# Layer 1 of the first two blocks in 256-token sets beside more attention, and all loops written out

## The chip, the cores and the metric

One Trainium2 chip, one core of it. The metric is the device time of the whole program in microseconds (us), from one launch. The engines are TensorE (PE; its weight loads are listed apart as PEld), VectorE (DVE), ScalarE (ACT), GpSimd (POOL), and SyncE (SP), which issues all transfers here. Work in PSUM is done in eight banks of 512 float32 columns.

## The reference

An attention with a decaying state, then two feed-forward layers. B = 4, H = 8, S = 768, D = 48; 3072 tokens of 384 values; d_ff is 1536 in layer 1 and 2048 in layer 2.

```python
for t in range(S):
    kt, vt, rt, wt = (k[:, :, t], v[:, :, t], r[:, :, t], w[:, :, t])
    cur = np.einsum('bhd,bhe->bhde', u[None] * kt, vt)
    y[:, :, t] = np.einsum('bhd,bhde->bhe', rt, state + cur)
    state = wt[:, :, :, None] * state + np.einsum('bhd,bhe->bhde', kt, vt)
...
gate = 1.0 / (1.0 + np.exp(-(x @ w_gate)))
val = x @ w_val
x = gate * val @ w_out
...
h = x @ w_in
g = np.where(h > 0.0, h, alpha * (np.exp(np.minimum(h, 0.0)) - 1.0))
out = g @ w_out
```

## The kernel before

The 768 time steps are six blocks of 128 (NB = 6), each of all four sequences, so of 512 tokens (TOK). Attention of a block is done in two halves (HALF), of two sequences each; q = 2n + hf numbers the twelve halves. A half goes through twelve stages (STAGES): transposes of w, k and r (Tw, Tk, Tr), six levels L1 to L6 at which the decays of ever longer runs are multiplied in, a transpose of k (KT), the output Y and the new state S. Each stage is two parts (b = 0, 1), one for each sequence, so a half has 24 parts. At a level TensorE multiplies (L544) what VectorE (`next_level_r`, L828) and GpSimd (`next_level_k`, L456) scaled for it; levels 1 to 3 have a masked copy on VectorE (L853), level 4 two sums (L861, L865), and levels 4 to 6 copies on ScalarE. The part of level i for sequence b waits for `next_level_r` of level i - 1 for the same b. The parts take the three banks 5 to 7 in turn, each waiting until the use three back has been read (`bank_free`). When both halves of a block have Y, a step XT transposes the result (L581), and ScalarE and VectorE copy it as a rounded high part xh and a low part xl (L888).

Layer 1 multiplies in three passes (high by high, high by low, low by high), in units called thirds. For each of the F1 = 12 tiles of d_ff there are the groups g (gate), v (value) and o (output), of three thirds each; a third is three matmuls (L606 for g and v, L615 for o) of 128 rows by 512 columns, in all 324 a block. After g ScalarE takes the sigmoid (L716); after v VectorE makes the product h (L907), ScalarE copies it rounded (hh, L669) and VectorE takes the rest (hl, L897), which o needs. The last two o groups (LATE) stand at the end.

The order is the same list for all engines, which each walk it in order. Block 0's attention comes first, alone (`FIRST`). Then `MIXED` is walked for n = 0 to 4: layer 1 of block n, with the 48 parts of block n + 1 spread over its 102 thirds, at the end XT of block n + 1 and LATE. For n = 1 to 4 it is a loop of the engines. `LAST` is layer 1 of block 5 alone. Then layer 2 follows for the six blocks (L631, L639), a loop too; it reads the result of layer 1 from a scratch in device memory (`store_x2`, `load_x2`).

The weights of layer 1 are 36 pieces of 128 x 384. Each is loaded into a ring of four (`raw_w1`, NR1), then ScalarE copies it rounded (L669, WS<-work) and VectorE takes the rest (L917); this is `split_w1`. Six are split in the second half of block 0 (`EARLY`), one more after each third third of layer 1 of block 0, until all 36 are. A group g waits for its tile's three pieces. SyncE's queue is in order: it waits for the ring, and for nat (w, k, r of a half) until level 4 of the half before has been done with it (`load_half` waits on d_shift).

Of the kernel before, what the change touches and what calls it, by code (L numbers as in the profile page):

```python
# [13 lines left out]
def build(nc, r, k, v, w, u, w_gate, w_val, w_out, w2_in, w2_out, out):  # L14
# [41 lines left out]

    def use_of(hf, name, i):

        return (HALF * ATT if name == "XT" else hf * ATT + 2 * STAGES.index(name)) + i

    def nth(hf, name, i):

        return use_of(hf, name, i) + 1

    ORDER = [(hf, name, i) for hf in range(HALF) for name in STAGES for i in range(2)] + \
            [(0, "XT", i) for i in range(KC)]
    AT = {use_of(*x): x for x in ORDER}

# [6 lines left out]
    THIRDS = [(*group, i) for group in GROUPS for i in range(3)]  # L75
    LATE = [("o", j, i) for j in (F1 - 2, F1 - 1) for i in range(3)]
    PARTS = [("a", hf, name, b) for hf in range(HALF) for name in STAGES for b in range(U)]
    XT = ("a", 0, "XT", 0)
    MIXED = []
    for i, third in enumerate(THIRDS):  # L80
        MIXED.append(third)
        MIXED += [PARTS[s] for s in range(len(PARTS)) if s * (len(THIRDS) - 3) // len(PARTS) == i]
    MIXED += [XT] + LATE
    FIRST = PARTS + [XT]
    LAST = THIRDS + LATE

    N1 = 3 * F1
    AHEAD = 6
    EARLY = [len(FIRST) // 2 + 10 + 2 * x for x in range(AHEAD)]
# [12 lines left out]
    with ctx:  # L102
# [35 lines left out]
        NR1 = 4  # L138
        raw_w1 = work[:, 0:NR1 * KC * P].rearrange("p (n f) -> p n f", n=NR1)
# [18 lines left out]
        w1_loaded = [sem(f"w1_loaded{i}") for i in range(NR1)]  # L158
        w2_loaded = [sem(f"w2_loaded{i}") for i in range(NR)]
        x2_stored, out_stored = sem("x2_stored"), sem("out_stored")  # L160
# [57 lines left out]
        def attn_bank(hf, name, i):  # L218
            return ATTN + use_of(hf, name, i) % NBK
# [791 lines left out]
```

## Time and profile before

| | |
|---|---|
| median of 3 runs | 1202.69 us (1201.72 to 1202.88) |
| the profiled execution, its span | 1203.3 us |
| PE busy | 1155.1 us, 96% |
| PEld busy | 1006.2 us, 84% |
| DVE busy | 669.5 us, 56% |
| ACT busy | 472.2 us, 39% |
| POOL busy | 295.5 us, 25% |
| block 0's attention, up to its XT | 90.8 us |
| layer 1 of block 0 with attention of block 1, XT to XT | 133.6 us |
| the same for later blocks | 121.8 us each |

A busy PE is not PE at its peak: a matmul's recorded length overlaps the next one's, so distances between starts tell its price. A weight load runs beside the matmul before it. "Idle before" of a row is how long that engine waited and for whom.

### The profile page before, as it was taken

How to read it: one execution, taken by the hardware profiler on the slowest of the kernel's cores; microseconds unless marked ns; L12 is line 12 of the kernel's file. 1: busy time of each engine (PE TensorE's matmuls, PEld its weight loads, DVE VectorE, ACT ScalarE, POOL GpSimd, SP SyncE). 2: the span in 40 equal slices, each digit the busy share in tenths (PEclk: the TensorE clock that was granted, in tenths of full speed). 3: DMA queues.
4: the chain of work that ended last, by engine and by line, in shares of the span. 5: the costliest groups of instructions: out<-in, count | busy, mean ns of one | idle time of the engine just before them, and what ended most of it. 6: DMA issues, size and time to landing. Idle time of an engine off the chain costs nothing.

```text
span 1203.3 us, 18133 instructions
## 1 busy us (share of the span) xinstructions
PE 1155.1 (96%) x6336; PEld 1006.2 (84%) x6336; DVE 669.5 (56%) x1044; ACT 472.2 (39%) x889; POOL 295.5 (25%) x290
## 2 busy tenths in 40 slices
PE   5778998999999999999999999999999999999999
PEld 4666777888888888888888888889999899899998
DVE  8777868494839393939393933354433334343433
ACT  2433444333333333333333333365544545454543
POOL 5563434143615351535153520000000000000000
PEclk9879998999999999999999999999999999999999
DMA  5451624122312231133204004220100101010000
GB/s 85 80 95 44 106 65 86 40 37 30 54 40 27 38 48 43 20 45 39 53 12 54 0 19 138 66 71 23 52 0 12 40 0 52 0 52 0 26 0 26
DMA packets 153413, 51.80 MB, mean 43 GB/s; under 512 B 126624, under 2 KB 148768, under 8 KB 153376
## 3 DMA queue, kind: packets, MB, share of 16 engines
q1 hardware_dynamic: 153376, 51.33, 21.0%
q8 instruction: 20, 0.33, 0.1%
q14 instruction: 17, 0.14, 0.0%
HBM read 41.88 MB, written 9.44 MB: 43 GB/s over the span
## 4 chain that ended last, share of the span: by engine, by line
PE 82%; DVE 11%; issue 4%; ACT 2%; DMA 0%; POOL 0%; DVEq 0%; SPq 0%; POOLq 0%; ACTq 0%
PE ps L606 21%; PE ps L639 17%; PE ps L631 16%; PE ps L615 10%; PE ps L544 7%; DVE RKW L828 6%; PE ps L560 3%; PE ps L534 3%; PE ps L565 2%; PE ps L573 2%; DVE hl L897 1%; DVE A L853 1%; DVE WS L917 1%; ACT RKW L669 1%; PE ps L581 1%
## 5 line engine op out<-in xcount | busy, mean ns | idle before, releaser
L606 PE MATMUL ps<-xh,WS 128*128 128x512 f32 x864 | 251.3, 408 | 1.6 <-DVE xl L888 1.6
L669 ACT ACTIVATE hh<-work 128x512 fp32r<-128x512 f32 x168 | 106.4, 633 | 287.5 <-DVE work L907 205.5
L544 PEld LDWEIGHTS ps<-RKW 128*128 128x128 f32 x1152 | 157.2, 203 | 59.1 <-DVE RKW L828 38.8
L544 PE MATMUL ps<-RKW 128*128 128x128 f32 x1152 | 167.6, 293 | 34.2 <-DVE RKW L828 34.0
L639 PE MATMUL ps<-WS,hh 128*128 128x384 f32 x768 | 198.0, 339 | 0.5 <-DVE hl L897 0.5
L828 DVE TENSOR_TENSOR RKW<-RKW,WL 64x256 f32<-64x256 f32 x288 | 186.1, 646 | 16.1 <-PE ps L544 13.7
L606 PEld LDWEIGHTS ps<-xh,WS 128*128 128x128 f32 x864 | 155.1, 190 | 30.7 <-issue 1.8
L897 DVE TENSOR_TENSOR hl<-work,hh 128x512 fp32r<-128x512 f32 x168 | 133.0, 791 | 85.3 <-ACT hh L669 84.3
L631 PE MATMUL ps<-xh,WS 128*128 128x512 f32 x576 | 164.2, 397 | 0.0
L615 PE MATMUL ps<-hh,WS 128*128 128x512 f32 x432 | 161.6, 411 | 0.4 <-DVE hl L897 0.3
L934 DVE SCALAR_TENSOR_TENSOR work<-work,ps 128x512 f32<-128x512 f32 x96 | 66.0, 688 | 172.2 <-ACT work L757 172.2
L456 POOL TENSOR_TENSOR RKW<-RKW,WL 128x256 f32<-128x256 f32 x144 | 111.0, 771 | 189.1 <-PE ps L544 189.1
L639 PEld LDWEIGHTS ps<-WS,hh 128*128 128x128 f32 x768 | 140.8, 188 | 8.7 <-DVE hl L897 1.0
L639 PE MATMUL ps<-WS,hl 128*128 128x384 f32 x384 | 129.9, 338 | 0.0
L606 PE MATMUL ps<-xl,WS 128*128 128x512 f32 x432 | 129.1, 407 | 0.0
L631 PEld LDWEIGHTS ps<-xh,WS 128*128 128x128 f32 x576 | 107.4, 188 | 18.8
L716 ACT ACTIVATE work<-ps 128x512 f32<-128x512 f32 x72 | 43.1, 599 | 155.8 <-PE ps L606 155.0
L755 ACT ACTIVATE work<-ps 128x512 f32<-128x512 f32 x96 | 57.2, 596 | 115.3 <-PE ps L631 115.3
L615 PEld LDWEIGHTS ps<-hh,WS 128*128 128x128 f32 x432 | 81.7, 189 | 17.3 <-DVE hl L897 1.3
L669 ACT ACTIVATE RKW<-ps 128x512 f32<-128x512 f32 (+1 forms) x120 | 70.9, 594 | 53.2 <-PE ps L534 52.8
L669 ACT ACTIVATE A<-ps 16x128 f32<-16x128 f32 (+2 forms) x168 | 57.9, 345 | 82.5 <-PE ps L544 81.0
L907 DVE TENSOR_TENSOR work<-work,ps 128x512 f32<-128x512 f32 x72 | 49.5, 688 | 72.6 <-PE ps L606 48.8
(67 smaller groups left out, 1324.7 us busy)
## 6 DMA issues: line engine op xcount, KB each, us to landing
nat<-in_w_dram SPq DMA_DIRECT2D x24, 192.0 KB, 3.7
nat<-in_k_dram SPq DMA_DIRECT2D x24, 192.0 KB, 4.8
nat<-in_r_dram SPq DMA_DIRECT2D x24, 192.0 KB, 5.2
V<-in_v_dram SPq DMA_DIRECT2D x24, 192.0 KB, 4.5
x_scratch<-work SPq DMA_DIRECT2D x6, 768.0 KB, 3.5
nat<-x_scratch SPq DMA_DIRECT2D x6, 768.0 KB, 5.2
out_dram<-Yt SPq DMA_DIRECT2D x5, 768.0 KB, 3.9
RKW<-in_moe_w_in_dram SPq DMA_DIRECT2D x16, 192.0 KB, 2.4
```

Of the source, the lines that this page charges most:

```text
L456: gp.tensor_tensor(Kb[:, :, :, 0, :], Kb[:, :, :, 0, :], Wb[:, :, :, 1].to_broadcast([P, PR, P // (2 * L), L]), ALU.mult).then_inc(p_k, 1)
L544: last = mm(bank[b][:, p * P:(p + 1) * P].rearrange("p (e i l) -> p e i l", e=2, l=L), K[:, g, :], Rb[:, :, :, 1, :], start=True, stop=True)
L606: last = mm(ps[:, VAL if val else GATE, :], gate_w(a, val, j, c), xp[b][:, c, :], start=(i == 0 and c == 0), stop=(i == 2 and c == KC - 1))
L615: last = mm(ps[:, ACC + i, :], down_w(a, j, i), hp[b][:, j % 2, :], start=(j == 0 and at == 0), stop=(j == F1 - 1 and at == 2))
L631: last = mm(ps[:, UP2 + j % 4, :], up2_w(a, j, c), xp[b][:, c, :], start=(i == 0 and c == 0), stop=(i == 2 and c == KC - 1))
L639: last = mm(ps[:, ACC2 + b, 0:HD], hp[ap][:, j % 2, b * P:(b + 1) * P], down2_w(wp, j), start=(j == 0 and i == 0), stop=(j == F2 - 1 and i ...
L669: return nc.scalar.activation(o, i, ACT.Copy)
L755: nc.scalar.activation(sig, ps[:, UP2 + j % 4, :], ACT.Relu, scale=-1.0).then_inc(a_relu, 1)
L828: last = tt(out_R, Rb, Wb[rows, :, :, 0].to_broadcast([HP, PR, P // (2 * L), L]), ALU.mult)
L897: tt(hl[:, j % 2, :], h, f32(hh[:, j % 2, :]), ALU.subtract).then_inc(d_lo, 1)
L907: tt(h, sig, ps[:, VAL, :], ALU.mult).then_inc(d_h, 1)
L934: nc.vector.scalar_tensor_tensor(h, sig, -1.0, ps[:, UP2 + j % 4, :], ALU.add, ALU.max).then_inc(d_elu, 1)
```

## The change

Layer 1 of blocks 0 and 1 is done in four sets of 256 tokens (two sequences, one half), the later blocks as before; `SETS` lists them, `cols(m)` gives a set's columns of the 512 in every tile and bank. A set 0 needs only half 0 of block 0, so its transposes (`transpose_x`, 6 for 12) stand after half 0, and half 1 of block 0 runs beside set 0. `STREAM` is all attention with the transposes, `PROGRAM` the whole order. Beside set 0 go the 24 parts of half 1 and the transposes for set 1; beside set 1 all 24 parts of half 2, the transposes and 8 parts of half 3 (`MORE`); beside set 2 the other 16, the transposes, and 16 of half 4; beside set 3 the other 8, half 5 whole and the transposes of block 2. From there the order is the former one.

A matmul of layer 1 in these sets has 256 columns for 512, so there are twice as many, 648 a block; the operations of ScalarE and VectorE on sig, h, hh, hl, xh, xl and x2 have 256 columns too and are twice as many. The six early weight pieces are split at levels 5, 6 and KT of half 0, the other 30 in set 0, again one after each third third. The first eight pieces are loaded ahead of half 1's inputs, two into unused space behind the ring and two into the idle half of Yt; after that the ring has four places. All loops are written out. Banks are given by the place of a use in `USES`; `x2_stored` is one semaphore a half.

```diff
+    HALVED = 2
+    TH = U * P
+    SETS = [(n, (hf,)) for n in range(HALVED) for hf in range(HALF)] + [(n, (0, 1)) for n in range(HALVED, NB)]
+    NS = len(SETS)
+    MORE = {1: 8, 2: 16}
+    def cols(m):
+
+        return slice(SETS[m][1][0] * TH, (SETS[m][1][-1] + 1) * TH)
...
+    PROGRAM = STREAM[:STREAM.index(("x", 0)) + 1]
+    done = len(PROGRAM)
+    phase = {}
+    for m in range(NS):
+        beside = STREAM[done:STREAM.index(("x", m + 1)) + 1 + MORE.get(m, 0)] if m + 1 < NS else []
+        done += len(beside)
+        phase.update({step: m for step in beside})
+        if beside and beside[-1][0] == "x" and SETS[m + 1][1] == (0, 1):
+            PROGRAM += spread(THIRDS[m], beside[:-1], len(THIRDS[m]) - 3) + [beside[-1]] + LATE[m]
+        else:
+            PROGRAM += spread(THIRDS[m], beside, len(THIRDS[m]) - 1) + LATE[m]
...
-    AHEAD = 6
-    EARLY = [len(FIRST) // 2 + 10 + 2 * x for x in range(AHEAD)]
+    EARLY = [("a", 0, name, b) for name in ("L5", "L6", "KT") for b in range(U)]
+    AHEAD = len(EARLY)
...
+        NR1, ONCE = 4, 4
+        raw_w1 = work[:, 0:(NR1 + 2) * KC * P].rearrange("p (n f) -> p n f", n=NR1 + 2)
+        raw_w1_y = Yt[:, G:2 * G].rearrange("p (n q) e d -> p n (q e d)", n=2)
...
-                    if x >= NR1:
-                        sp.wait_ge(d_wlo, x - NR1 + 1)
-                    dst = raw_w1[:, x % NR1, :]
+                    if x >= NR1 + ONCE:
+                        sp.wait_ge(d_wlo, x - (NR1 + ONCE if x < 2 * NR1 + ONCE else NR1) + 1)
+                    dst = w1_raw(x)
...
+            at = [2 * NR1 + ONCE] + [min(N1, NR1 + split_until(("a", 1, name, 1))) for name in ("L4", "Y")] + [N1]
             load_w1(at[0], at[1])
-            load_half(1, 1)
-            load_v(1, 1)
+            load_half(2)
+            load_v(2)
             load_w1(at[1], at[2])
...
+            def transpose_x(m):
+                n, halves = SETS[m]
+                pe.wait_ge(d_y, 2 * (HALF * n + halves[-1] + 1))
+                for c in range(KC):
+                    bank_free("x", m, c)
+                    for b in range(halves[0] * U, (halves[-1] + 1) * U):
+                        last = nc.tensor.transpose(ps[:, bank_of("x", m, c), b * P:(b + 1) * P],
+                                                   o_sb[:, b, c * P:(c + 1) * P], ident[:])
+                    last.then_inc(s_att, 1)
...
                     for c in range(KC):
-                        last = mm(ps[:, VAL if val else GATE, :], gate_w(a, val, j, c), xp[b][:, c, :],
+                        last = mm(ps[:, VAL if val else GATE, t], gate_w(a, val, j, c), xp[b][:, c, t],
                                   start=(i == 0 and c == 0), stop=(i == 2 and c == KC - 1))
...
-            with pe.Fori(1, NB - 1) as i:
-                mixed(i)
-            for step in LAST:
-                layer1(NB - 1, *step)
-            with pe.Fori(0, NB) as i:
+            for step in PROGRAM:
+                if step[0] == "a":
+                    attention(*step[1:])
+                elif step[0] == "x":
+                    transpose_x(step[1])
+                else:
+                    layer1(*step[1:])
+            for n in range(NB):
                 for step in STEPS2:
-                    layer2(i, *step)
+                    layer2(n, *step)
```

TensorE's order where layer 1 begins. Before, after both halves (L573 is S, L581 the transposes to x, L534 Tw and Tk of block 1):

```order
L573 MATMUL ps<-V,RKW 128x96 x8
L581 MATMUL ps<-ident,Yt 128x128 x12
L606 MATMUL ps<-xh,WS 128x512 x3
L534 MATMUL ps<-ident,nat 128x128 x4
L606 MATMUL ps<-xl,WS 128x512 x3
L606 MATMUL ps<-xh,WS 128x512 x3
L534 MATMUL ps<-ident,nat 128x128 x4
```

Now, after half 0 alone (L588 is S, L532 the transposes, L550 Tw of half 1 of block 0, L614 the gate and value matmuls):

```order
L588 MATMUL ps<-V,RKW 128x96 x8
L532 MATMUL ps<-ident,Yt 128x128 x6
L614 MATMUL ps<-xh,WS 128x256 x3
L550 MATMUL ps<-ident,nat 128x128 x4
L614 MATMUL ps<-xl,WS 128x256 x3
L614 MATMUL ps<-xh,WS 128x256 x6
L614 MATMUL ps<-xl,WS 128x256 x3
L550 MATMUL ps<-ident,nat 128x128 x4
```

The transposes to x moved ahead by one half, and a part stands after every four thirds instead of after every second one.

VectorE's order at levels 1 and 2 beside the first layer-1 work. Before, in block 1 (L828 `next_level_r`, L853 the masked copy, L897 the low part, L917 a weight split):

```order
L828 TENSOR_TENSOR RKW<-RKW,WL 64x4x32x2 x2
L853 COPY_PREDICATED A<-masks,ps 128x256x2
L897 TENSOR_TENSOR hl<-work,hh 128x512
L917 TENSOR_TENSOR WS<-work,WS 128x384
L828 TENSOR_TENSOR RKW<-RKW,WL 64x4x32x2 x2
L853 COPY_PREDICATED A<-masks,ps 128x256x2
L828 TENSOR_TENSOR RKW<-RKW,WL 64x4x16x4 x2
L853 COPY_PREDICATED A<-masks,ps 128x128x4
```

Now, in half 1 beside set 0 (L817, L842, L888, L909 are the same four, L899 the product h):

```order
L817 TENSOR_TENSOR RKW<-RKW,WL 64x4x32x2 x2
L842 COPY_PREDICATED A<-masks,ps 128x256x2
L909 TENSOR_TENSOR WS<-work,WS 128x384
L817 TENSOR_TENSOR RKW<-RKW,WL 64x4x32x2 x2
L842 COPY_PREDICATED A<-masks,ps 128x256x2
L899 TENSOR_TENSOR work<-work,ps 128x256
L909 TENSOR_TENSOR WS<-work,WS 128x384
L888 TENSOR_TENSOR hl<-work,hh 128x256
L909 TENSOR_TENSOR WS<-work,WS 128x384
L817 TENSOR_TENSOR RKW<-RKW,WL 64x4x16x4 x2
L842 COPY_PREDICATED A<-masks,ps 128x128x4
```

Between level 1 and level 2 of the first sequence there were one split and one layer-1 operation; now there are three splits and two layer-1 operations of half the width.

## Rows read from the trace of the kernel before

**Rows 1.** The page: busy, 40 slices in tenths, and the chain by engine.

```profile
PE 1155.1 (96%) x6336; PEld 1006.2 (84%) x6336; DVE 669.5 (56%) x1044; ACT 472.2 (39%) x889; POOL 295.5 (25%) x290
DVE  8777868494839393939393933354433334343433
...
PE 82%; DVE 11%; issue 4%; ACT 2%; DMA 0%; POOL 0%; DVEq 0%; SPq 0%; POOLq 0%; ACTq 0%
```

**Rows 2.** Windows by stage: length, busy PE PEld DVE ACT POOL, PEclk, DMA, GB/s.

```profile
48.50:90.83 42.33, 31.07 (x194) 28.13 (x193) 34.65 (x57) 14.79 (x34) 23.92 (x23) 0.80 0.43 74
90.83:224.46 133.63, 122.25 (x705) 102.50 (x704) 100.82 (x158) 52.12 (x112) 49.59 (x46) 0.97 0.36 71
224.46:346.29 121.83, 120.71 (x721) 103.93 (x720) 78.06 (x127) 41.43 (x86) 48.51 (x46) 1.00 0.23 40
```

**Rows 3.** Windows, the six levels of halves 0, 2, 3 and 4.

```profile
15.50:39.71 24.21, 16.94 (x96) 15.73 (x97) 22.70 (x36) 4.95 (x15) 14.27 (x15) 0.86 0.26 44
...
106.94:141.21 34.27, 29.99 (x172) 24.38 (x173) 30.29 (x51) 12.92 (x32) 15.99 (x17) 1.00 0.38 72
168.59:205.96 37.37, 32.48 (x172) 27.11 (x171) 32.78 (x51) 13.59 (x33) 16.07 (x17) 0.91 0.43 80
241.69:271.26 29.57, 29.10 (x172) 24.52 (x171) 27.84 (x42) 9.82 (x24) 15.06 (x17) 1.00 0.31 41
```

**Rows 4.** Timeline of PEld: start, length of the group, form, count.

```profile
748.01 1.36 PEld L606 LDWEIGHTS ps<-xh,WS 128*128 128x128 f32 x6
749.42 0.66 PEld L606 LDWEIGHTS ps<-xl,WS 128*128 128x128 f32 x3
...
902.35 0.19 PEld L639 LDWEIGHTS ps<-WS,hl 128*128 128x128 f32 x1
...
904.11 0.60 PEld L631 LDWEIGHTS ps<-xh,WS 128*128 128x128 f32 x3
...
86.28 1.87 PEld L560 LDWEIGHTS ps<-V,A 128*128 128x128 f32 x16
...
88.07 0.97 PEld L565 LDWEIGHTS ps<-ST,RKW 128*128 128x128 f32 x8
```

**Rows 5.** Timeline at the ends of half 0, of block 0, and at block 2's first dense matmul.

```profile
48.48 1.78 PE L534 MATMUL ps<-ident,nat 128*128 128x128 f32 x12
...
90.72 0.91 PEld L581 LDWEIGHTS ps<-ident,Yt 128*128 128x128 f32 x8
90.83 1.72 PE L581 MATMUL ps<-ident,Yt 128*128 128x128 f32 x12
...
94.13 0.94 PE L606 MATMUL ps<-xh,WS 128*128 128x512 f32 x3 [1.58 <-DVE xl L888]
...
351.82 0.86 PE L606 MATMUL ps<-xh,WS 128*128 128x512 f32 x3
```

**Rows 6.** Timeline in block 1's first half, levels 1 and 2, with releasers.

```profile
110.12 0.56 DVE L917 TENSOR_TENSOR WS<-work,WS 128x384 fp32r<-128x384 f32 x1 [1.11 <-ACT WS L669]
...
112.78 0.97 PEld L544 LDWEIGHTS ps<-RKW 128*128 128x128 f32 x8 [1.39 <-DVE RKW L828]
```

**Rows 7.** Groups by form, block 2's layer 1 (346.29 to 468.12), VectorE and ScalarE.

```profile
L893 DVE TENSOR_TENSOR WL<-RKW 128x512 f32<-128x512 f32 x2 | 1.4, 692 | 8.6 <-ACT RKW L669 8.6
L893 DVE TENSOR_TENSOR WL<-WL 128x256 f32<-128x256 f32 x2 | 0.8, 424 | 0.1
...
L669 ACT ACTIVATE A<-ps 32x256 f32<-32x256 f32 x8 | 3.0, 375 | 2.6 <-PE ps L544 2.6
```

**Rows 8.** A window of L917 alone, half 2's levels; its group, 90.83 to 224.46.

```profile
106.94:141.21 34.27, 5.95 (x9) 1.00 0.38 72
...
L917 DVE TENSOR_TENSOR WS<-work,WS 128x384 fp32r<-128x384 f32 x30 | 22.4, 750 | 17.6 <-ACT WS L669 17.5
```

**Rows 9.** Timeline of SyncE's issues around the loads of a half.

```profile
134.11 0.99 SPq L244 DMA_DIRECT2D nat<-in_w_dram  x2
...
141.47 1.11 SPq L280 DMA_DIRECT2D work<-in_moe_w_val_dram  x1
```

More of the change, by code:

```diff
@@ L74, in build, with spread, splits @@
         GROUPS += [("g", j), ("v", j)] + ([("o", j - 1)] if 1 <= j < F1 - 1 else [])
[L75 to L85, printed above, removed]
-    N1 = 3 * F1
-    AHEAD = 6
-    EARLY = [len(FIRST) // 2 + 10 + 2 * x for x in range(AHEAD)]
+    THIRDS = [[("d", m, *group, i) for group in GROUPS for i in range(3)] for m in range(NS)]
+    LATE = [[("d", m, "o", j, i) for j in (F1 - 2, F1 - 1) for i in range(3)] for m in range(NS)]
+    def spread(dense, parts, room):
+        steps = []
+        for i, third in enumerate(dense):
+            steps.append(third)
+            steps += [parts[s] for s in range(len(parts)) if s * room // len(parts) == i]
+        return steps
+    PROGRAM = STREAM[:STREAM.index(("x", 0)) + 1]
[9 more added lines that the diff above has]
+            PROGRAM += spread(THIRDS[m], beside, len(THIRDS[m]) - 1) + LATE[m]
+    assert done == len(STREAM)
+    N1 = 3 * F1
+    EARLY = [("a", 0, name, b) for name in ("L5", "L6", "KT") for b in range(U)]
+    AHEAD = len(EARLY)
+    def splits(step):
+        return step in EARLY or (step[:2] == ("d", 0) and step[-1] == 2)
+    SPLIT1 = {step: x for x, step in enumerate([step for step in PROGRAM if splits(step)][:N1])}
+    SPLIT2 = {("d", NS - 1, "v", j + 1, 2): j for j in range(F1 - 2)}
+    assert len(SPLIT1) == N1
     DOWNS = F2 - 1 + B
@@ L332, in _ @@
-            load_shift(v, 1, 0)
+            load_v(0)
+            load_shift(v, 0)
+            load_w1(0, NR1 + ONCE)
+            load_half(1)
+            load_v(1)
+            load_w1(NR1 + ONCE, 2 * NR1 + ONCE)
+            load_shift(k, 1)
+            load_shift(v, 1)
             def split_until(step):
-                return AHEAD + sum(x[0] != "a" and x[-1] == 2 for x in MIXED[:MIXED.index(step)])
-            at = [NR1 + AHEAD] + [NR1 + split_until(("a", hf, name, 1)) for hf, name in ((0, "L4"), (0, "Y"), (1, "L4"))] + [N1]
+                return sum(PROGRAM.index(x) < PROGRAM.index(step) for x in SPLIT1)
@@ L374, in _ @@
                 load_w2(j)
-            store_x2(NB - 1)
-            sp.wait_ge(x2_stored, 16 * (NB + 1))
-            with sp.Fori(0, NB - 1) as i:
-                load_x2(i + 1)
-                store_out(i)
+            store_x2(NS - 1)
+            for n in range(NB - 1):
+                load_x2(n + 1)
+                store_out(n)
             for b in range(B):
@@ L705, in attention, with transpose_x, layer1 @@
                         last.then_inc(a_rp, 1)
-                elif name == "XT":
-                    for c in range(KC):
-                        act.wait_ge(s_att, ATT_BLK * n + nth(hf, name, c))
-                        copy(xh[:, c, :], ps[:, attn_bank(hf, name, c), :]).then_inc(a_xhi, 1)
-            def layer1(n, kind, j, third):
+            def transpose_x(m):
+                t = cols(m)
+                for c in range(KC):
+                    act.wait_ge(s_att, count("x", m, c))
+                    copy(xh[:, c, t], ps[:, bank_of("x", m, c), t]).then_inc(a_xhi, 1)
+            def layer1(m, kind, j, third):
+                t = cols(m)
                 if third < 2:
```

473 lines of the change are left out of this document (197 added, 276 removed).

## The prediction

> **What bounds the kernel now.** I read the busy row and the slices first [rows 1]: TensorE is busy 96% of the span, and VectorE, 56% in all, is at seven to eight tenths in the first seven slices (some 210 us). The chain is 82% TensorE and 11% VectorE [rows 1]. The windows by stage show why [rows 2]: from 48.50 to 90.83 us, the second half of block 0 alone, TensorE shows work for 31 of 42 us; the block that follows (layer 1 of block 0 with attention of block 1) takes 133.63 us, and the next 121.83 us, with TensorE busy 120.71. That gives two things to win: the 42.3 us in which the second half stands alone, and the 11.8 us by which the first mixed block is longer.
>
> What the waits are is seen in the windows over the six levels of one half [rows 3]. In the half that runs first (15.50 to 39.71) they take 24.21 us with VectorE busy 22.70. In block 1's two halves they take 34.27 and 37.37 us with VectorE busy 30.29 and 32.78; in the first of block 2's 29.57, where TensorE is busy 29.10. So levels are VectorE's while weights are being split, and just about even later.
>
> **The price of a matmul.** Busy times of matmuls overlap, so I take the distance between starts of weight loads, one per matmul [rows 4]. 512 columns: six loads from 748.01, the next at 749.42, 0.235 each; over a long stretch 0.232. 384 columns: ten from 902.35 to 904.11, 0.176. Attention's float32 ones of 48 columns (each runs as two instructions): sixteen from 86.28 to 88.07, 0.112; its matmuls of 128 columns also stand at 0.112 (eight loads end 0.97 after the first starts [rows 6]). From 512 to 384 the step is 0.056 per 128 columns, so **256 columns cost 0.176 - 0.056 = 0.120**, a price that before has no row for. Its bounds: 0.112, the pace of the shortest pairs (gain), and 0.190, the mean duration of one weight load, if each had to end before the next matmul. I take 0.120, since the 48-column loads also last 0.19 [rows 4] and follow at 0.112.
>
> With these, TensorE's own work is: one half of attention, 32 transposes at 0.109 (eight from 90.72 show 0.91 [rows 5]) and 160 other executed pairs (96 of levels, 64 of the Y and S stages) at 0.112, 21.4 us; layer 1 of a block, 324 matmuls, 75.2 us at 512 columns and 2 x 324 x 0.120 = 77.8 us in two sets; so 38.9 us a set and **+2.6 us a block, +5.2 us** in all. A transpose step to the next layer is 0.65 us for a set and 1.3 us for a block.
>
> **Up to the first set.** The half alone ends at 48.48 [rows 5]. Six weight pieces are now split at its levels 5, 6 and KT, which stood in the second half before. Six splits of 0.56 [rows 6] would be 3.3 us, if VectorE were the bound throughout; it is busy 94% of the levels [rows 3], but the stage KT, where two of the six fall, waits for others. So between 2.2 and 3.3, and little is certain of the two: I take 2.3, and 50.8. From the transposes to the first dense matmul were 94.13 - 90.83 = 3.3 us [rows 5]; with six transposes for twelve (-0.65) and copies of 256 columns (0.42 for 0.69 on VectorE [rows 7], as much again on ScalarE), 2.2 us: first dense matmul at 53.0.
>
> **Set 0, with the second half and 30 splits beside.** TensorE's work is 38.9 + 21.4 + 0.65 = 61.0 us. The code puts a half's 24 parts over 101 thirds of layer 1, so the six levels (12 parts) span 48.5 thirds: 48.5 x 3 x 0.120 + 12 x 0.896 = 28.2 us of TensorE. VectorE in the same stretch: attention alone 22.7 us in the half alone [rows 3]; in half 2 30.29 less nine splits of 5.95 [rows 8] and six products and low parts of 0.69, 20.2; I take 21.7. Sixteen splits, one after every third third, at 0.69, between 5.95/9 = 0.66 and the group's mean of 0.750 [rows 8]: 11.0. Five products and five low parts at 0.42 and 0.46 (a 256-column operation is 0.424 where 512 take 0.692, ScalarE's 256-element copy 0.375 [rows 7]): 4.7. Each split behind a product waits for ScalarE, which copies h first and the weight piece second; before, 1.11 us [rows 6], now 0.85 with the shorter copy, times 5.4: 4.6. Other idle 0.7. Sum **42.7 us against 28.2: +14.5 us**. The same sum gives before's 34.27 (30.29 busy + 3.3 on ScalarE + 0.7). The three transpose stages ahead come to 14 us against 11.4; one part's lead absorbs some: +1.8. KT, Y and S (16.8 us of TensorE, 12.8 of VectorE) hide everything. Set 0 is 77.3 us, and ends at 130.3.
>
> **Sets 1 to 3, with 1.33 halves each.** TensorE's work is 3 x 38.9 + 4 x 21.4 + 2 x 0.65 + 1.3 = 204.9 us. Parts stand 3.06 thirds apart, so six levels are 24.0 us of TensorE. VectorE has 21.7 + 3.6 (eight layer-1 operations) + 1.5 idle as in the half alone = 26.8: +2.9 a half. Bounds: 25.3 with no idle (+1.4), and 25.3/0.88 = 28.8 (+4.8), 0.88 being busy over length in block 1's levels [rows 3]. The masked levels and level 4 have the most work in a row, so I take 3.5, **+14 us** for four halves. Three banks go round, and a transpose step is followed by the next T after three thirds (1.1 us) where before the late down projections stood between: about 0.5 us twice and 0.5 at the first whole block, +1.5.
>
> **The sum.** The first dense matmul of block 2 stood at 351.82 [rows 5]; after that the order is before's, unrolled. Now: 53.0 + 77.3 + 204.9 + 14 + 1.5 = 350.7. Difference -1.1 us. In the profiled execution that is 1203.3 - 1.1 = 1202.2; its span stands 0.6 us over the median 1202.69, so 1201.6. Loops gone: a pass of the loop has TensorE busy 120.71 of 121.83 us [rows 2], and the levels' waits make up most of the rest, so nothing is counted. The saved 42.3 us are eaten by 21.4 + 0.65 of work that must still be done, 5.2 of shorter matmuls, 2.3 of splits and some 13 to 16 of waits beyond the former.
>
> **TensorE's rule.** The rows show 0.232 for 512 columns and 0.176 for 384 [rows 4]. The Trainium skill (TensorE: Matmul & The Clock Gate, Back-to-back issue gap) gives 262 cycles for 256 columns, 0.109 us at 2.4 GHz. By that the price would be below mine and at the attention pairs' floor; it is the third rival. The same table gives 518 cycles, 0.216, for 512, which the trace contradicts by 0.016.
>
> **The rivals.**
> First, slower: VectorE's levels in sets 1 to 3 behave like block 1's (0.88 busy at the higher density, waits falling between in-order operations) and set 0's splits take their mean of 0.750 [rows 8]: 4 x (4.8 - 3.5) = 5.2, 16 x 0.06 = 1.0, and the three heavy levels and level 4 (4.4, 4.4, 4.4, 4.8 of VectorE plus 0.6 of layer 1 each, 20.6, against 15.9 of TensorE) cannot lend to the light ones, up to another 1 a half: 10 us, 1211. For it: the gaps before level matmuls [rows 6]. Against: block 2's first half, whose levels wait 0.5 us where the same count of the heavy levels gives 1.5 to 2. It decides if levels in sets 1 to 3 last over 28.5 us.
> Second, slower: the weight load shows. At 0.190 a pair, 1296 x 0.070 = 91 us, of which VectorE-bound stretches (some 590 matmuls) hide part: about 1260. Against: 48-column loads at 0.112.
> Third, faster: 0.112 for 256 columns. Only some 640 of 1296 matmuls are outside VectorE-bound levels: 640 x 0.008 = 5 us, 1196.
> Fourth, faster: the levels of sets 1 to 3 fit (+1.4 a half, -8.4) and splits run at the 0.56 of an undisturbed one [rows 6] (-2): 1191.
> A fifth cost is in the queue: SyncE issues the next half's eight loads ahead of the next weight piece, 134.11 to 141.47 [rows 9], 7.4 us, plus some 3.5 to land, against four pieces in the ring. At 2.6 us a piece the ring lasts 10.6 us, so I count nothing; at TensorE's own pace (1.75) it would cost 4 us, and that is in the range. TensorE's granted clock was 0.86 in the mean over the first half's levels and 0.91 over those of block 1's second half [rows 3], so part of either stood at the lower level, 1.2 GHz; with TensorE two thirds busy in set 0's levels this may come again, hidden by VectorE.
>
> **Chances.** My sum 0.47 (1197 to 1206), first rival 0.20, second 0.03, third 0.14, fourth 0.16. The measurement tells a change from none at about 0.2%, 2.4 us: 1200.3 to 1205.1. Of my sum 0.14 lies below, 0.25 within, 0.08 above. Faster 0.14 + 0.14 + 0.16 = 0.44, same 0.25, slower 0.31. Range 1190 to 1211.
>
> **What will show it.** The second half's first transposes beside dense matmuls at about 53 us; weight loads of 256-column matmuls 0.120 apart; set 0's six levels 43 us long with VectorE over 85% busy; the following four 27.5 us; the transposes of block 2 near 348. Wrong if 256-column pairs are off 0.120 by more than 0.008, if ScalarE waits for a weight DMA in set 0, or if levels in sets 1 to 3 show no VectorE wait.

## The result and the profile after

The changed kernel takes 1218.24 us (median of 4 runs, 1212.75 to 1222.15) against 1202.79 (1201.72 to 1205.14): ratio 1.0125, 95% interval 1.0097 to 1.0152. It is **slower by 1.25%**, 15.5 us between the medians, where I forecast 1201.6 and had 1211 as the upper end. Its executions lie at 1213 to 1214 and at 1222; the long ones have the lower mean granted clock (0.979 and 0.983, the short ones 0.987 and 0.99).

The profiled execution is one of the short ones: 1214.37 us, span 1212.7. Its page, busy, slices and chain:

```profile
span 1212.7 us, 17955 instructions
...
PE 1158.1 (96%) x6984; PEld 1041.3 (86%) x6984; DVE 672.6 (55%) x1098; ACT 481.0 (40%) x949; POOL 289.1 (24%) x290
...
DVE  8886576775767484748474843344333334343433
...
PE 79%; DVE 14%; issue 4%; ACT 2%; DMA 1%; POOL 0%; SPq 0%; DVEq 0%; POOLq 0%
```

Beside [rows 1], TensorE has the same share, and the chain has moved from TensorE to VectorE by three points. The windows by stage (length, busy PE PEld DVE ACT POOL, PEclk, DMA, GB/s) are the sets 0 to 3, from first dense matmul to first dense matmul, and the first whole block:

```profile
52.32:135.10 82.78, 68.75 (x522) 65.95 (x523) 57.43 (x107) 34.63 (x85) 24.07 (x23) 0.94 0.37 82
135.10:208.30 73.20, 67.03 (x565) 65.97 (x563) 50.91 (x94) 27.63 (x66) 30.69 (x30) 0.98 0.21 33
208.30:284.00 75.70, 69.81 (x587) 68.18 (x587) 56.26 (x100) 26.39 (x70) 31.90 (x33) 0.99 0.29 45
284.00:362.42 78.42, 74.77 (x619) 72.97 (x617) 47.77 (x87) 27.38 (x66) 29.70 (x29) 0.98 0.29 44
362.42:483.90 121.48, 120.77 (x721) 104.03 (x721) 77.40 (x127) 40.83 (x86) 48.16 (x46) 1.00 0.22 37
```

Block 2's first dense matmul stands at 362.42, where before's stood at 351.82 [rows 5]: 10.6 us later. From there on the changed kernel needs 850.3 us of its span, before 851.5. So all of the loss lies in the four sets, and two of my terms are missed: set 0 has 82.78 us for 77.3, and sets 1 to 3 have 227.3 for 220.4.

What TensorE waited for in sets 1 to 3 (waits of the trace: us in total, times, longest):

```profile
PE ps L560 <- DVE RKW L817: 9.0, 9, 2.1
PE ps L623 <- DVE hl L888: 6.0, 3, 3.5
```

The same waits counted at the weight loads, which come first and so show the whole gap:

```profile
PEld ps L560 <- DVE RKW L817: 12.8, 16, 2.3
PEld ps L623 <- DVE hl L888: 6.6, 3, 3.7
```

The first row of each is the wait at the levels that I had sized. The second isn't in my sum at all: the down projection waits for hl, the low part of the product. With two small ones, of 0.6 and 0.2 us, the weight loads wait 20.2 us in the three sets.

### The profile page after: what moved, and what is told of

It reads as the page before. It is cut to its first block, busy times and chain, and to the rows that moved or that the text cites. A ratio compares the mean times of both kernels' runs of the same rounds, so it can differ in the third digit from the quotient of the medians.

```text
span 1212.7 us, 17955 instructions
## 1 busy us (share of the span) xinstructions
PE 1158.1 (96%) x6984; PEld 1041.3 (86%) x6984; DVE 672.6 (55%) x1098; ACT 481.0 (40%) x949; POOL 289.1 (24%) x290
## 4 chain that ended last, share of the span: by engine, by line
PE 79%; DVE 14%; issue 4%; ACT 2%; DMA 1%; POOL 0%; SPq 0%; DVEq 0%; POOLq 0%
PE ps L614 20%; PE ps L647 17%; PE ps L639 16%; PE ps L623 9%; DVE RKW L817 8%; PE ps L560 6%; PE ps L575 3%; PE ps L550 3%; DVE A L842 2%; PE ps L580 2%; PE ps L588 2%; ACT RKW L670 1%; DVE WS L909 1%; DVE hl L888 1%; DVE work L899 1%
## 5 line engine op out<-in xcount | busy, mean ns | idle before, releaser
L614 PE MATMUL ps<-xh,WS 128*128 128x256 f32 (+1 forms) x1152 | 265.2, 350 | 6.7 <-DVE WS L909 3.3
L670 ACT ACTIVATE hh<-work 128x512 fp32r<-128x512 f32 (+1 forms) x192 | 111.3, 580 | 340.0 <-DVE work L899 255.0
L614 PEld LDWEIGHTS ps<-xh,WS 128*128 128x128 f32 x1152 | 184.4, 192 | 28.2 <-DVE WS L909 3.9
L817 DVE TENSOR_TENSOR RKW<-RKW,WL 64x256 f32<-64x256 f32 x288 | 186.1, 646 | 20.5 <-PE ps L560 18.1
L623 PE MATMUL ps<-hh,WS 128*128 128x256 f32 (+1 forms) x576 | 176.1, 355 | 12.1 <-DVE hl L888 11.9
L888 DVE TENSOR_TENSOR hl<-work,hh 128x512 fp32r<-128x512 f32 (+1 forms) x192 | 136.6, 712 | 91.8 <-ACT hh L670 90.6
L639 PE MATMUL ps<-xh,WS 128*128 128x512 f32 x576 | 164.1, 397 | 0.0
L614 PE MATMUL ps<-xl,WS 128*128 128x256 f32 (+1 forms) x576 | 140.3, 352 | 0.0
L623 PEld LDWEIGHTS ps<-hh,WS 128*128 128x128 f32 x576 | 105.2, 191 | 25.2 <-DVE hl L888 14.4
L614 PEld LDWEIGHTS ps<-xl,WS 128*128 128x128 f32 x576 | 93.8, 193 | 9.6
L721 ACT ACTIVATE work<-ps 128x256 f32<-128x256 f32 (+1 forms) x96 | 47.0, 490 | 138.1 <-PE ps L614 137.1
L623 PE MATMUL ps<-hl,WS 128*128 128x256 f32 (+1 forms) x288 | 98.0, 340 | 0.0
L899 DVE TENSOR_TENSOR work<-work,ps 128x256 f32<-128x256 f32 (+1 forms) x96 | 53.2, 554 | 67.1 <-PE ps L614 47.4
```

The lines of the kernel that those rows point to most:

```text
L614: last = mm(ps[:, VAL if val else GATE, t], gate_w(a, val, j, c), xp[b][:, c, t], start=(i == 0 and c == 0), stop=(i == 2 and c == KC - 1))
L623: last = mm(ps[:, ACC + i, t], down_w(a, j, i), hp[b][:, j % 2, t], start=(j == 0 and at == 0), stop=(j == F1 - 1 and at == 2))
L639: last = mm(ps[:, UP2 + j % 4, :], up2_w(a, j, c), xp[b][:, c, :], start=(i == 0 and c == 0), stop=(i == 2 and c == KC - 1))
L670: return nc.scalar.activation(o, i, ACT.Copy)
L817: last = tt(out_R, Rb, Wb[rows, :, :, 0].to_broadcast([HP, PR, P // (2 * L), L]), ALU.mult)
L888: tt(hl[:, j % 2, t], h[:, t], f32(hh[:, j % 2, t]), ALU.subtract).then_inc(d_lo, 1)
```

## The experiments

Set lengths in the table go from first dense matmul to first dense matmul, of one profiled execution each; "start" is where the first dense matmul stands in it. "Lowest" is the shortest execution; "ratio" is to the kernel before on the same chip. "Same, again" is the changed kernel once more, whose median stands 0.12 us from the first.

| kernel | median us | lowest us | ratio (95%) | start | set 0 | set 1 | set 2 | set 3 |
|---|---|---|---|---|---|---|---|---|
| after | 1218.24 | 1212.75 | 1.0125 (1.0097 to 1.0152) | 52.32 | 82.78 | 73.20 | 75.70 | 78.42 |
| same, again | 1218.12 | 1213.69 | 1.0128 (1.0095 to 1.0161) | 52.30 | 85.70 | 73.22 | 76.24 | 78.21 |
| weights first | 1215.85 | 1213.10 | 1.0104 (1.0084 to 1.0123) | 58.32 | 86.62 | | | |
| earlier set ends | 1214.22 | 1212.67 | 1.0116 (1.0082 to 1.015) | 51.54 | 82.69 | 74.71 | 74.92 | 76.85 |
| weighted spread | 1210.41 | 1207.90 | 1.0048 (1.0019 to 1.0076) | 59.27 | 86.39 | 73.58 | 71.67 | 74.51 |
| block 0 alone in sets | 1207.90 | 1206.14 | 1.0032 (1.0003 to 1.006) | 52.46 | 84.49 | 98.85 | | |
| that, weighted | 1206.34 | 1205.37 | 1.0018 (0.9992 to 1.0045) | 53.07 | 85.74 | 94.42 | | |
| low parts on GpSimd | 1217.32 | 1216.34 | 1.0101 (1.0067 to 1.0135) | 52.67 | 85.95 | | | |
| weight copy first | 1210.82 | 1208.88 | 1.0068 (1.0039 to 1.0098) | 58.81 | 79.57 | | | |
| without two GpSimd products | 1192.59 | 1189.76 | 0.9929 (0.9897 to 0.996) | 49.58 | 79.93 | 68.84 | 72.95 | 73.80 |
| before, unrolled | 1201.40 | 1198.35 | 0.9994 (0.9967 to 1.0021) | 94.52 | | | | |
| before, unrolled, copy first | 1194.80 | 1194.23 | 0.9929 (0.9904 to 0.9954) | 92.99 | | | | |
| block 0 in sets, all edits | 1198.48 | 1192.92 | 0.995 (0.9933 to 0.9966) | 58.89 | 73.02 | 95.04 | | |

The starts fall into two groups. In four traces the first dense matmul stands at 58.3 to 59.3 us, and each of them has one stretch of 17.1 us at 1.2 GHz (from 38.08 to 55.15 in "weights first"), while half 0 is still alone; in the others with sets it stands at 49.6 to 53.1. No edit acts there in "weights first", "weighted spread" and "weight copy first", so these 6 to 7 us belong to the execution and not to the edit. A median depends on how many executions have that stretch. So I compare medians with the lowest execution beside them, and an edit's effect is what both show.

**The same kernel again.** No edit.

> The changed kernel once more, with a second profile, as the base of the others. Its executions so far stood near 1213 and near 1222 us. If the chip's clock is the cause of the two levels, a slow execution shows a lower mean clock and a fast one 0.99; ratio to before 1.008 to 1.016.

Set 0 took 85.70 us instead of 82.78 in the same program. The window in which they part, late in set 0 (columns as above):

```profile
112.04:125.00 12.96, 12.43 (x68) 12.13 (x68) 5.68 (x11) 4.74 (x12) 0.64 (x1) 0.60 0.35 92
```

TensorE is busy throughout at a granted clock of 0.60, so most of this stretch stood at 1.2 GHz. VectorE is busy less than half of it, so there the clock isn't hidden. The expectation held: the longest execution, 1221.59 us, has 0.983, and the ratio lies in its range. In all, set 0 had 17.1 us at the lower level against 10.2 in the first trace, and is 2.9 us longer.

**All weight pieces ahead of half 2's inputs.**

```diff
-            load_w1(at[0], at[1])
+            load_w1(at[0], at[3])
             load_half(2)
             load_v(2)
-            load_w1(at[1], at[2])
...
-            load_w1(at[2], at[3])
```

> All 36 weight pieces of layer 1 are issued ahead of half 2's inputs, so no weight piece queues behind eight input loads. Theory A (weights starve): ScalarE's 3.2 us wait for a weight DMA and TensorE's 4.2 us gap near 110 us are gone, set 0 takes about 79 us instead of 82.8, and the time falls 3 to 4 us. Rival B (VectorE is the bound of set 0 anyway): the gap goes but set 0 stays within 1 us of 82.8. Rival C: half 2's inputs now come late and the first transposes of set 1 wait, up to 5 us.

ScalarE's wait for a weight transfer (3.2 us once in the changed kernel, shown further down) is gone. The median falls by 2.3 us, the lowest execution doesn't fall (1213.10 for 1212.75), and this profile's set 0 is longer, not shorter, with 20.5 us at the lower clock. Behind the levels TensorE still waits 1.97 us for hl, where it was 3.90, and then 1.10 for a weight piece of VectorE. So the 3 to 4 us of theory A aren't there: most of the wait stays when the transfer is in time. The trace shows more of the clock. Both windows hold the same 86 matmuls from 38.10 to the first dense one, the changed kernel first:

```profile
38.10:52.32 14.22, 10.45 (x86) 9.64 (x87) 13.44 (x21) 6.44 (x15) 6.95 (x6) 1.00 1.06 175
```
```profile
38.10:58.32 20.22, 17.89 (x86) 17.05 (x87) 11.52 (x20) 5.54 (x13) 6.46 (x5) 0.58 0.69 116
```

At a clock of 0.58 TensorE becomes the bound and the end of half 0 takes 6.0 us more. VectorE's busy time falls from 13.44 to 11.52 us, so the longer stretch is not its doing.

**Parts of sets 1 and 2 end seven thirds earlier**, so that the down projections at the set's end have no attention beside them.

```diff
-            PROGRAM += spread(THIRDS[m], beside, len(THIRDS[m]) - 1) + LATE[m]
+            PROGRAM += spread(THIRDS[m], beside, len(THIRDS[m]) - (1 if m == 0 or not beside else 8)) + LATE[m]
```

> In sets 1 and 2 the last part of attention stands 7 thirds earlier, so no level work of VectorE stands between the last value group and the last product and low part. Theory A (attention in the tail delays the last product): the waits of the last down projection for hl, 3.5 us at 206 and 2 us at 282, fall to under 1 us each, time down 3 to 5 us. Rival B (the levels need VectorE all the same): the wait moves to the next level matmul, time within 1 us.

TensorE's waits over sets 1 to 3:

```profile
PE ps L560 <- DVE RKW L817: 10.0, 14, 1.6
PE ps L623 <- DVE hl L888: 0.8, 2, 0.4
```

The waits for hl nearly go, from 6.0 to 0.8, as they should. But 3.1 us of waits for the product appear (work, L899) and the levels, packed more closely, wait 10.0 for 9.0: the sum falls from 15.0 to 13.9, the three sets from 227.3 to 226.5. At the weight loads nothing is gained: 15.3 us for RKW, 4.0 for the product and 1.2 for hl are 20.5, for 20.2, and the lowest execution stays (1212.67 for 1212.75). This is rival B: VectorE is late, and where the order lets TensorE meet it is second to that.

**The kernel before with its loops written out.**

```diff
-            with pe.Fori(1, NB - 1) as i:
+            for i in range(1, NB - 1):
```
(and so for each loop of each engine)

> The kernel before with its loops written out and nothing else changed. In the changed kernel the later blocks took 121.4 us instead of 121.83. Theory A (loops cost a little at the levels): the four looped blocks are 0.4 to 0.5 us shorter each, time down 1.5 to 2 us, ratio 0.998 to 0.999. Rival B: the 0.45 us came from the sets ahead, and this kernel is within 0.5 us of before.

The first block keeps 135.87 us, a later one has 121.39 instead of 121.83, as in the changed kernel (121.48). The loops were worth 0.4 us a block, and are no part of the loss. In the block the result stands as theory A had it; in the whole time, 1201.40 for 1202.79 with the ratio's interval on both sides of 1, it can't be told.

**A weighted spread.** Each part takes room by its weight on VectorE: 20 for levels 1 to 4, 12 for levels 5 and 6, 8 for transposes, 2 for Y and 4 for S. Two parts of half 4 also move from set 2 to set 3.

```diff
-    MORE = {1: 8, 2: 16}
+    MORE = {1: 8, 2: 14}
...
+        return 20 if name in ("L1", "L2", "L3", "L4") else 12 if name[0] == "L" else {"Y": 2, "S": 4}.get(name, 8)
...
-            steps += [parts[s] for s in range(len(parts)) if s * room // len(parts) == i]
+            steps += [parts[s] for s in range(len(parts)) if (sum(map(weight, parts[:s])) * room) // sum(map(weight, parts)) == i]
```

> The same sets, but the attention beside them is spread by weight: five shares of dense thirds after a part of levels 1 to 4, three after levels 5 and 6, two after a transpose part, one or less after Y and S; 14 parts instead of 16 of half 4 go beside set 2. Theory A (TensorE waits because VectorE's work of a half is bunched in levels 1 to 4, not because of its total): level waits in sets 1 to 3 fall from about 15 us to under 5, and set 0 keeps most of its wait; the time falls 8 to 12 us. Rival B (VectorE's total and its in-order chain product, rounded copy, low part set the pace): waits move to the down projections, time within 3 us of the changed kernel.

Sets 2 and 3 lose 4.0 and 3.9 us, set 1 nothing; the median falls by 7.7, the lowest execution by 4.9. TensorE's waits for RKW over the three sets are 5.1 us for 9.0; at the weight loads all waits are 14.4 us for 20.2. Of set 0, 86.39 us with 17.1 at the lower clock, this execution tells nothing. The result lies between the two theories: a good part of the waits was bunching, and more than 5 us of them stay. An even spread by number is thus a cost of its own: the levels come faster than VectorE does them, and Y and S leave it idle.

**Block 0 alone in sets**, with the even spread and with the weighted one.

```diff
-    HALVED = 2
+    HALVED = 1
-    MORE = {1: 8, 2: 16}
+    MORE = {}
```

> Only block 0 in 256-token sets; block 1 whole again, so both halves of block 1's attention (48 parts) stand beside set 1. It does one part of the change alone: starting layer 1 early. Theory A (sets of block 1 bring only waits and short matmuls, starting early is what wins): set 1 takes 88 to 95 us, block 1's layer 1 begins at 223 to 230 us (229.98 before), blocks then 121.4 us, time 1196 to 1202. Rival B (48 parts beside one set wait for VectorE at every level, 6 levels of 4 us each against 2.8 of TensorE): set 1 over 98 us, time 1206 or more.

> The same with the weighted spread beside both sets of block 0. If bunching is what costs (theory A of the weighted run), 4 to 8 us less than the run without weights; if VectorE's total binds beside set 1 (56 us of attention and 10 of layer 1 in some 85), within 2 us of it.

Set 1, with a whole block of attention beside 324 matmuls of 256 columns, takes 98.85 us, and 94.42 weighted. Block 1's first dense matmul stands at 235.80, before's at 229.98. At block 2 the loss is 5.5 us (357.30 for 351.82), half of the changed kernel's 10.6, and the time is what rival B named. Weighting gives set 1 4.4 us and takes 1.3 in set 0, so the time falls by 1.6 us at most, where 4 to 8 were expected.

**Low parts of 30 weight pieces on GpSimd** instead of VectorE.

```diff
-            for step in STREAM:
+            for step in PROGRAM:
...
+                if step in SPLIT1 and step not in EARLY:
+                    x = SPLIT1[step]
+                    pool.wait_ge(a_whi, x + 1)
+                    gp.tensor_tensor(w1_piece(x, 1), w1_raw(x), f32(w1_piece(x, 0)), ALU.subtract).then_inc(d_wlo, 1)
...
-                if step in SPLIT1:
+                if step in SPLIT1 and step in EARLY:
```

> The changed kernel with the low parts of the 30 weight pieces of set 0 taken by GpSimd instead of VectorE. Theory A (set 0 is bound by VectorE's sum of attention, splits and waits for ScalarE): set 0 falls from 82.8 to 68 to 74 us. Rival B (set 0 is bound by the chain of levels and by the loads): within 3 us of 82.8. Rival C: GpSimd holds VectorE's port for each of its 30 operations and set 0 gets longer, 85 us or more.

VectorE loses 30 operations and set 0 is no shorter. The group of VectorE's level products in set 0 (count | busy, mean ns of one | idle before), the changed kernel and this one:

```profile
L817 DVE TENSOR_TENSOR RKW<-RKW,WL 64x256 f32<-64x256 f32 x24 | 14.0, 583 | 0.2
```
```profile
L821 DVE TENSOR_TENSOR RKW<-RKW,WL 64x256 f32<-64x256 f32 x24 | 20.3, 845 | 1.1 <-PE ps L564 1.0
```

The same instruction takes 845 ns instead of 583. GpSimd, now busy 54.78 us in set 0 for 24.07, holds VectorE up. The 85.95 us are rival C's figure, but 20.5 of them are at the lower clock, so how much GpSimd adds to the set isn't told apart.

**Without two GpSimd products.** This kernel leaves out most of two products: with u it does one head of eight for each sequence, of the shifted keys with r one of sixteen. Its result is thus not the reference's; all else is unchanged.

```diff
-                        mine = own[:, b * H:(b + 1) * H, :]
+                        mine = own[:, b * H:b * H + 1, :]
...
-                    gp.tensor_tensor(near, near, heads(nat[:, 0]), ALU.mult).then_inc(p_shift, 1)
+                    gp.tensor_tensor(near[:, 0:1, :], near[:, 0:1, :], heads(nat[:, 0])[:, 0:1, :], ALU.mult).then_inc(p_shift, 1)
```

> Leaves out most of two of GpSimd's products (own terms times u, and the shifted k times r): they work on one head of sixteen, so the diagonal terms of the result are not the reference's. VectorE's level operations take 0.42 us alone and 0.77 when a GpSimd operation of over 0.5 us runs beside. Theory A (GpSimd's long products at levels 1 and 2 hold VectorE and make the level waits of the dense sets): the second level stage of sets 1 to 3 falls from 6.7 to about 4.5 us, sets 1 to 3 together 6 to 10 us shorter, whole blocks 0.5 to 1 us each. Rival B (VectorE's own work is the bound, GpSimd only overlaps): under 2 us in all.

The products go into sums of VectorE, not into a matmul, and VectorE's list of waits names GpSimd neither with them nor without. So what changes at the levels is VectorE's company. The level products over sets 1 to 3, the changed kernel and this one:

```profile
L817 DVE TENSOR_TENSOR RKW<-RKW,WL 64x256 f32<-64x256 f32 x96 | 64.6, 673 | 9.8 <-PE ps L560 9.0
```
```profile
L817 DVE TENSOR_TENSOR RKW<-RKW,WL 64x256 f32<-64x256 f32 x96 | 52.7, 549 | 9.1 <-PE ps L560 8.3
```

and TensorE's waits there, in this kernel:

```profile
PE ps L623 <- DVE hl L888: 4.1, 3, 2.0
PE ps L560 <- DVE RKW L817: 2.8, 3, 1.3
```

11.9 us of VectorE's time on unchanged instructions go, TensorE's waits for RKW fall from 9.0 to 2.8 us, and sets 1 to 3 from 227.3 to 215.6. At the weight loads all waits fall by 10.1 us, from 20.2 to 10.1. That is the largest single effect found, and over theory A's. A whole block gains only 1.8 us (119.68), a set 3.9 in the mean: the same hindrance costs four times as much per column where the order is dense. But the kernel before has the same products, and none of its runs leaves them out. So this shows what GpSimd costs the changed kernel, not that it makes the difference between the two.

**ScalarE copies the weight piece ahead of h**, where both fall on one third.

```diff
+                elif step in SPLIT1 and step[2] == "v":
+                    split_w1(SPLIT1[step])
+                    layer1(*step[1:])
...
-                if step in SPLIT1:
+                if step in SPLIT1 and step[2] != "v":
```

> The changed kernel with ScalarE's order turned at the twelve value groups of set 0: the weight piece's rounded copy first, the copy of h second. Theory A (VectorE's idle time behind the product, 0.85 us a group as predicted, is part of what stretches set 0): VectorE's wait for ScalarE's weight copies falls from 16.3 us to under 8, set 0 falls by 4 to 8 us from 82.8 to 85.7. Rival B (set 0 is held by ScalarE's copy of h, which now comes 0.5 us later, and by TensorE's lower clock): set 0 within 2 us.

Set 0 takes 79.57 us for 82.78 and 85.70; VectorE's waits for ScalarE's weight copy in it fall from 16.3 to 12.2 us, not to under 8. Both traces have 10.2 us of set 0 at the lower clock, so the 3.2 us are the order's. The median is 7.4 us lower, the lowest execution 3.9: more of the median isn't shown to be the edit's. With this order in **the kernel before, unrolled**:

> The kernel before, loops written out, with the same turned order of ScalarE in its first layer-1 block. If VectorE's 17.5 us of waiting for weight copies there is on the path (theory A), that block falls from 135.9 to 130 to 132 us and the time to 1196 to 1198; if the levels' own work is the bound (rival B), within 1.5 us of 1201.4.

Block 0's layer 1 takes 128.04 us for 135.87. VectorE's wait for the weight copy there:

```profile
DVE WS L921 <- ACT WS L669: 9.0, 6, 4.0
```

It was 17.5 [rows 8], and TensorE's waits for RKW fall from 9.4 to 4.7 us. Theory A is borne out, by more than it named; 6.8 us of the 135.87 stood at the lower clock and 3.4 of the 128.04, which is at most 1.7 us of the gain. By its median this is the fastest kernel that computes all: 1194.80 us, 0.7% below before, at an interval clear of 1.

**All edits together**: block 0 alone in sets, the weighted spread in all blocks (whole blocks with weights of their own), all weights first, the weight copy first.

> Block 0 alone in sets, the weighted spread in all blocks (whole blocks with milder weights), weight pieces issued first, and ScalarE's order turned. By theory A of those runs: set 0 77 to 80 us, set 1 about 92, whole blocks 120.5 instead of 121.4: 1192 to 1199, below the kernel before. Rival B (each wait moves on to the next one): 1203 to 1207.

1198.48 us, below before but 3.7 above the last, inside theory A's range. Set 0 is down to 73.02 us. The profiled execution, 1198.77 us, has the stretch of 17.1 us at 1.2 GHz ahead of set 0:

```profile
38.10:58.89 20.79, 17.94 (x87) 17.09 (x87) 12.06 (x20) 6.05 (x15) 6.93 (x6) 0.59 0.65 118
```

Its block 1 begins at 226.95 us, in the kernel of the last experiment at 221.03; with the start at 52.3 it would be some 220.4, an estimate. Seven of the eight executions lie at 1198.1 to 1199.6 and one, with a mean clock of 0.993, at 1192.92, below all four of the last experiment (1194.23 to 1196.18). Its whole blocks take 121.12 us, 0.3 less than there, which isn't the sets' doing. So with these edits the sets about break even with the second half alone, and what decides is how often the clock falls ahead of them. That the other six have the same stretch is not shown.

## Why the prediction was wrong, step by step

**The price of 256 columns was sound.** Three, three and six weight loads in set 0 (start, length, form, count):

```profile
106.02 0.42 PEld L614 LDWEIGHTS ps<-xh,WS 128*128 128x128 f32 x3
106.37 0.43 PEld L614 LDWEIGHTS ps<-xl,WS 128*128 128x128 f32 x3
106.73 0.78 PEld L614 LDWEIGHTS ps<-xh,WS 128*128 128x128 f32 x6
```

0.35 us and 0.36 for three: 0.117 to 0.120 apart, elsewhere down to 0.115, for my 0.120. Over sets 1 to 3 the mean is 0.118. The third rival had the sign and a quarter of its size, 0.002 instead of 0.008. The second, with 0.190, is out.

**Up to the first set**: 52.32 for 53.0, and half 0 done at 49.80 for 50.8. This held, but only at full clock; the same matmuls took 6.0 us more where the clock fell.

**Set 0: 82.78 for 77.3.** The term I had taken most trouble over stands: its six levels, 67.18 to 107.56, take 40.38 us, predicted 42.7, with VectorE busy 33.84 of them (84%) where I named over 85%. (Five products and five low parts at 0.42 and 0.46 are 4.4 us, not 4.7; that is the sum for the 5.4 groups of the term behind it.) The stages ahead take 14.86 us for 13.2. The step that failed is "KT, Y and S hide everything", with "I count nothing" for the ring: from 107.56 to 135.10 are 27.54 us where my sum leaves 21.4. Right behind the levels, in the changed kernel:

```profile
110.06 1.12 ACT L670 ACTIVATE WS<-work 128x384 fp32r<-128x384 f32 x2 [3.20 <-DMA work<-in_moe_w_gate_dram]
...
112.78 0.39 PE L623 MATMUL ps<-hh,WS 128*128 128x256 f32 x1 [3.90 <-DVE hl L888]
```

ScalarE waits 3.20 us for a weight piece, which I had named as a sign of being wrong. VectorE waits for ScalarE, hl is late and TensorE stands still for 3.90 us. The ring ran dry by about as much as I had worked out for TensorE's own pace and then not counted. But mending the transfers alone left 1.97 us of that wait and a new one of 1.10, and the lowest execution where it was: VectorE is also late there. In all TensorE waits 4.3 us in this stretch, and 3.4 us of it stand at 1.2 GHz, worth at most 1.7; together that is about the 6.1. The other failed step is "this may come again, hidden by VectorE": 6.9 us more at the lower clock came with 2.9 us more of set 0 in the repetition. It isn't hidden once the levels are over.

**Sets 1 to 3: 227.3 for 220.4.** TensorE's own work is some 202.9 us at 0.118 a pair, so 24.4 us are waits and slow stretches where I had 15.5. Of these the weight loads wait 20.2 us for VectorE where I had 14; 6.8 us stand at the lower clock, worth at most 3.4, where I had none; the 1.5 for banks don't show, and the rest isn't told apart. Half 2's levels, 144.71 to 171.57, take 26.86 us, within 0.7 of the 27.5 named; half 5's, 313.86 to 343.29, take 29.43, so by my own mark the first rival decides there. (Those of halves 3 and 4 stand across the end of a set and can't be compared.) The waits at the levels, 12.8 us, are about my 14. The step that failed is **"+14 us for four halves" as all that VectorE costs**: I averaged it over a half's six levels and looked for its waits there alone, while 6.6 us came at hl. The end of set 1:

```profile
200.94 2.44 POOL L443 TENSOR_TENSOR nat<-nat,ub 128x384 f32<-128x384 f32 x2
...
201.27 2.40 DVE L817 TENSOR_TENSOR RKW<-RKW,WL 64x256 f32<-64x256 f32 x2
...
203.70 1.29 DVE L842 COPY_PREDICATED A<-masks,ps 128x512 f32<-128x512 int32 x1
...
204.80 0.45 DVE L899 TENSOR_TENSOR work<-work,ps 128x256 f32<-128x256 f32 x1
...
205.73 0.43 DVE L888 TENSOR_TENSOR hl<-work,hh 128x256 fp32r<-128x256 f32 x1 [0.48 <-ACT hh L670]
206.21 0.58 PE L623 MATMUL ps<-hh,WS 128*128 128x256 f32 x1 [3.48 <-DVE hl L888]
```

Because eight parts of half 3 run ahead into set 1, a level's two products (2.40 us, beside two of GpSimd) and a masked copy (1.29) stand on VectorE between the last value group and the product h. Then come h, ScalarE's hh, and hl, and TensorE has nothing left but the late down projection: 3.48 us. Set 2's end costs 2.0 more in the same way. I had looked at the set ends only for banks and transposes. Nor is the place itself the cause, since with earlier set ends the 20.2 us of waits became 20.5 elsewhere: what was too small is VectorE's share in the three sets as a whole.

**The duration of a level product.** I took VectorE's work from the levels of halves 0 and 2. In the changed kernel the products take 673 ns in the mean over sets 1 to 3. Which of them are long is seen on the timeline:

```profile
260.49 2.17 POOL L443 TENSOR_TENSOR nat<-nat,ub 128x384 f32<-128x384 f32 x2
260.85 2.10 DVE L817 TENSOR_TENSOR RKW<-RKW,WL 64x256 f32<-64x256 f32 x2
...
264.47 2.68 DVE L817 TENSOR_TENSOR RKW<-RKW,WL 64x256 f32<-64x256 f32 x2
264.87 1.99 POOL L447 TENSOR_TENSOR shift<-shift,nat 128x768 f32<-128x768 f32 x1
...
267.20 0.97 PEld L560 LDWEIGHTS ps<-RKW 128*128 128x128 f32 x8 [1.82 <-DVE RKW L817]
```

Two pairs of products take 2.10 and 2.68 us beside GpSimd products, against 0.84 a pair alone, and TensorE's weight load then waits 1.82 us. Of the level products of the whole kernel, the 139 with no long GpSimd operation beside have a mean of 416 ns, 197 others 773. This is not new in the changed kernel, though. Before, 126 have 418 ns and 210 have 751; the mean is 671 ns in half 0's levels, and in block 2's:

```profile
L828 DVE TENSOR_TENSOR RKW<-RKW,WL 64x256 f32<-64x256 f32 x48 | 30.6, 638 | 3.2 <-PE ps L544 2.8
```

So the length was in my 21.7 us, and is no step that failed; VectorE is busy 26.19 and 26.60 us at the levels of halves 2 and 5, where I had 25.3. What differs is how little TensorE has to do meanwhile: 24.0 us over six levels by my sum, for 29.10 busy in half 4 before [rows 3].

**The whole blocks.** I counted nothing for the loops; they gave 0.44 us a block (121.83 to 121.39).

**The rivals.** The first (VectorE's levels in sets 1 to 3, 1211) was the right mechanism and fell short: its 10 us didn't contain the set ends, the ring and the clock. The fourth, 1191, is near the kernel with GpSimd's products left out (1192.59), by chance: its terms were others. In the profiled execution the terms close: 351.82 before, 350.7 predicted; -0.7 at the start, +5.5 in set 0, +6.9 in sets 1 to 3 give 362.4. The rest of the program gained 1.2. The remaining 4 us between this execution and the median go with the clock. The long executions of the changed kernel itself have no trace. But three profiled executions with an edit that acts later, 1217.38 to 1224.33 us, all have the stretch of 17.1 us at 1.2 GHz and begin set 0 6.0 to 7.0 us late, and the unprofiled ones of 1222 us have a mean clock as low as theirs (0.979 and 0.983, against 0.978 to 0.985). Between lowest executions the loss is 11.0 us (1212.75 for 1201.72), near the profile's.

**What stays open.** The split of sets 1 to 3's loss between order and GpSimd isn't clean, since weighting saves 7.5 us there and leaving out the products 11.7, and both act on the same waits; they weren't run together. No run leaves the products out of the kernel before, so it stays open how much of GpSimd's cost is the change's. Nor is it known why the clock falls in one execution of a program and not in another, and whether the changed order makes it fall more often.

## What to carry to other kernels

Filling a stretch in which TensorE is idle pays only by what the engine behind the idleness can spare: here 42.3 us of a half alone were won, and VectorE, not TensorE, had to absorb the second half, so all of it came back, as TensorE's own work and as waits. Before moving work, go through the busiest follower's queue between two dependent dense steps, instead of averaging it over a stage, and spread the moved work by the follower's busy time, not by number. And look for an order inside one engine that delays another: turning two ScalarE copies round gave some 4 us in the changed kernel and 4 to 7 in the one before (lowest executions and medians), with no work saved. Before a few us of a median are put down to an edit, see whether a slow stretch of the clock ahead of it differs.

## What the hardware showed

- VectorE's product of 64 x 256 float32 values from two SBUF operands takes 0.42 us alone and up to 2.04 us beside a GpSimd product. 30 more operations on GpSimd raised its mean from 583 to 845 ns. The Trainium skill (SBUF — State Buffer, SBUF: two separate sides) says that a VectorE operation with two SBUF inputs and a GpSimd one that reads SBUF exclude each other for a whole instruction. The trace agrees: each of the four VectorE products shown above, two from 260.85 and two from 264.47 us, ends 0.27 to 0.29 us after a GpSimd product does, whatever its length (0.72 to 1.94 us).
- TensorE's granted clock fell to 1.2 GHz in stretches of 3.4 to 17 us after stretches in which TensorE had waited (at 205.69, within the wait of 3.48 us at the end of set 1), in some executions of a program and not in others. Where TensorE was the bound in them, the same 86 matmuls took 20.22 us for 14.22.
- Pairs of weight load and matmul follow at 0.115 to 0.120 us for 256 columns, hardly above the 0.112 for 48 [rows 4]. The Trainium skill (TensorE: Matmul & The Clock Gate, Back-to-back issue gap) gives 262 cycles, 0.109 us at 2.4 GHz, for matmuls that have no weight load between them; the trace stands 0.006 to 0.011 above.
